# First three attention steps skewed by one level with their decays on VectorE, and each later step prepared one group earlier

## The reference

```python
def _attn_ref(q, k, v, alpha):            # (4, 8, 768, 48) each
    for t in range(S):
        state = alpha[:, :, t, :, None] * state + einsum('bhd,bhe->bhde', k[:, :, t], v[:, :, t])
        y[:, :, t] = einsum('bhd,bhde->bhe', q[:, :, t], state)
def _moe_ref(x, w_gate, w_val, w_out):    # x (3072, 384), d_ff 1536
    return (sigmoid(x @ w_gate) * (x @ w_val)) @ w_out
def _moe2_ref(x, domain_probs, w1, w2):   # 4 experts, F 1024
    p = domain_probs / (domain_probs.sum(-1, keepdims=True) + 1e-09)
    out = sum over e of p[:, e:e + 1] * (maximum(x @ w1[e], 0) @ w2[e])
```

## Time and profile before

| | |
|---|---|
| median of 3 runs | 1492.99 us (1491.99 to 1493.7) |
| profiled execution | 1493.83 us, span 1492.0 us |
| TensorE busy | 1438.6 us, 96% of the span |
| VectorE, ScalarE, GpSimd busy | 620.4, 501.0, 597.8 us |
| first dense matmul | 65.81 us after the span's start |

### The profile page before, as it was taken

One profiled execution on the slowest core, in us unless ns is written; L12 is line 12 of the kernel. 1 busy time (PEld: TensorE's weight loads), 2 busy tenths in 40 slices (PEclk: granted clock), 3 DMA queues, 4 the chain that ended last, 5 costly groups with the idle time before them and its releaser, 6 DMA issues.

```text
span 1492.0 us, 25792 instructions
## 1 busy us (share of the span) xinstructions
PE 1438.6 (96%) x10296; PEld 1327.3 (89%) x10296; DVE 620.4 (42%) x908; ACT 501.0 (34%) x975; POOL 597.8 (40%) x570
## 2 busy tenths in 40 slices
PE   3799999999999999999999999999999999999999
PEld 3688999898999898999999999999999999999998
DVE  8766654646455555312333333333333333333332
ACT  5554444545445445322222222222222222222220
POOL 7666454544444535254423413323234133242120
PEclk9999999999999999999999999999999999999999
DMA  6512122112121212100001001010010010100011
GB/s 229 188 51 102 51 84 70 68 67 70 66 88 52 93 60 83 43 22 22 0 1 43 0 1 43 0 43 1 1 42 0 0 42 0 42 0 0 19 44 63
DMA packets 31115, 70.70 MB, mean 47 GB/s; under 512 B 5168, under 2 KB 14128, under 8 KB 31024
## 3 DMA queue, kind: packets, MB, share of 16 engines
q1 hardware_dynamic: 31024, 69.43, 13.6%
HBM read 64.70 MB, written 4.72 MB: 47 GB/s over the span
## 4 chain that ended last, share of the span: by engine, by line
PE 89%; DVE 5%; issue 2%; POOL 2%; ACT 1%; DMA 1%; SPq 0%; DVEq 0%; ACTq 0%; POOLq 0%
PE PS L637 27%; PE PS L627 27%; PE PS L583 19%; PE PS L593 9%; PE PS L531 3%; PE PS L554 1%; DVE KQ L861 1%; PE PS L550 1%; ACT QX L738 1%; PE PS L534 1%; DVE near L866 1%; DMA V<-in_v 1%; DVE KQ L846 1%; DVE TOT L855 1%; DMA KQ<-in_qk 0%
## 5 line engine op out<-in xcount | busy, mean ns | idle before, releaser
L1094 POOL TENSOR_TENSOR XS_0l<-x2T,XS_0h 128x1536 fp32r<-128x1536 f32 x24 | 84.4, 3516 | 261.5 <-ACT XS_0h L781 261.5
L985 DVE SCALAR_TENSOR_TENSOR acc<-PS,prob,acc 128x384 f32<-128x384 f32 x192 | 118.7, 618 | 160.5 <-PE PS L637 160.5
L1094 POOL TENSOR_TENSOR XS_1l<-x2T,XS_1h 128x1536 fp32r<-128x1536 f32 x23 | 80.7, 3509 | 250.6 <-ACT XS_1h L781 250.6
L738 ACT ACTIVATE QX<-KQ 48x256 f32<-48x256 f32 x288 | 120.8, 419 | 139.5 <-DVE KQ L846 102.9
L820 ACT ACTIVATE H_1h<-PS 128x512 fp32r<-128x512 f32 x96 | 57.4, 598 | 309.9 <-PE PS L627 309.9
L820 ACT ACTIVATE H_0h<-PS 128x512 fp32r<-128x512 f32 x96 | 57.2, 598 | 297.3 <-PE PS L627 297.2
L846 DVE TENSOR_TENSOR KQ<-KQ,TOT 112x512 f32<-112x512 f32 (+1 forms) x144 | 126.9, 891 | 66.2 <-PE PS L531 37.7
L993 DVE SCALAR_TENSOR_TENSOR H_1l<-PS,H_1h 128x512 fp32r<-128x512 f32 x96 | 66.4, 691 | 195.8 <-ACT H_1h L820 195.8
L993 DVE SCALAR_TENSOR_TENSOR H_0l<-PS,H_0h 128x512 fp32r<-128x512 f32 x96 | 66.1, 691 | 187.4 <-ACT H_0h L820 187.4
L531 PE MATMUL PS<-QX,KQ 112*64 112x64 f32 x1920 | 86.7, 237 | 41.2 <-ACT QX L738 36.2
L531 PEld LDWEIGHTS PS<-QX,KQ 112*64 112x64 f32 x1920 | 73.2, 148 | 56.8 <-issue 27.9
(11 more groups left out here) (152 smaller groups left out, 4137.1 us busy)
## 6 DMA issues: line engine op xcount, KB each, us to landing
row<-in_rows SPq DMA_DIRECT2D x24, 768.0 KB, 4.3
KQ<-in_qk SPq DMA_DIRECT2D x24, 448.0 KB, 4.1
V<-in_v SPq DMA_DIRECT2D x24, 384.0 KB, 4.8
rawA<-in_w SPq DMA_DIRECT2D x8, 768.0 KB, 4.8
rawB<-in_w SPq DMA_DIRECT2D x8, 768.0 KB, 6.4
A<-in_alpha SPq DMA_DIRECT2D x24, 224.0 KB, 2.7
out_y<-acc SPq DMA_DIRECT2D x5, 768.0 KB, 3.5
raw<-in_w_gate SPq DMA_DIRECT2D x3, 768.0 KB, 8.4
```

The source lines that it names most:

```text
L738: done = nc.scalar.activation(QX[p][rows, :, g, :].rearrange("d a (n t) -> d a n t", t=2 << level), right, ACT.Copy)
L985: dve.scalar_tensor_tensor(out=acc[:, n, :], in0=PS[:, result_banks[u], 0:DM], scalar=weight, in1=acc[:, n, :], op0=ALU.mult, op1=ALU.add) ...
L1094: nc.gpsimd.tensor_tensor(XS[c % 2][1][:], x2T[:, :, at:at + T2], XS[c % 2][0][:].bitcast(F32), ALU.subtract).then_inc(xsl_ready, 1)
```

## The change

It does five things.

1. `FIRST` is a wave: step 1 runs one level behind step 0, and step 2 one behind step 1; before, all three ran the same level in turn.
2. The decays of these three steps are made by VectorE (`first_decays`, a `tensor_reduce` with multiplication over pairs, after each level) in PSUM banks 0, 1 and 2, which no one uses yet. GpSimd no longer makes them.
3. Steps 1 and 2 have row buffers of their own, so that all rows are loaded at the start; before, each load waited for the near terms of the step ahead.
4. The work on weight pieces moves: the low parts of pieces 3 to 5 are made by VectorE in tile 0, in ten parts, one behind each of the groups 0 to 9; the preparation of step 3 stands in slot 0 of tile 0.
5. In the slot tables a step's PREP stands two slots ahead of its level 0, not one, and in tile 0 all attention tasks stand two slots later.

The core of the diff, the tables and their use:

```diff
     def at(n):
-        return (n + lead) * ATT_GROUPS // count
+        return 2 + 2 * (n + lead) if first_tile else n * ATT_GROUPS // (4 * STEPS_T)
+    if first_tile:
+        slots[0].append((PREP, 0, 0))
...
             if 0 <= level < LEVELS:
                 tasks.append((LVL, j, level))
             if level == 0:
-                slots[at(n) - 1].append((PREP, j, 0))
+                slots[at(n) - 2].append((PREP, j, 0))
...
-FIRST = [(LVL, j, n) for n in range(LEVELS) for j in range(STEPS_T)]
...
+for n in range(LEVELS + STEPS_T + 2):
+    FIRST += [(LVL, j, n - j) for j in range(STEPS_T) if 0 <= n - j < LEVELS]
+    for j in range(STEPS_T):
+        if n - j == LEVELS:
+            FIRST += [(YOUT, j, 0), (STATE, j, 0)]
+        if n - j == LEVELS - 1:
+            FIRST.append((TRK, j, 0))
+        if n - j == LEVELS + 1:
+            FIRST.append((TRX, j, 0))
...
+        def tot_of(i, sc, h):
+            if not is_first(i, sc):
+                return TOT[buffer_of(i, sc)][h]
+            at = 2 * PAIRS * (HC - C // h)
+            return PS[:, sc, at:at + PAIRS * C // h].rearrange("r (a m) -> r a m", a=PAIRS)
...
+            def first_decays(sc, n):
+                if n:
+                    dve.wait_ge(*decays_done(0, sc, n))
+                tot = tot_of(0, sc, 2 << n)[0:R].rearrange("p a (n w) -> p a n w", w=2)
+                dve.tensor_reduce(tot_of(0, sc, 4 << n)[0:R], tot, AX.X, ALU.mult).then_inc(first_decay[sc], 1)
...
-            for j in range(STEPS_T):
-                decays(0, j)
             near_products(0, 0)
+            near_products(0, 1)
+            low_raw1(0)
             near_terms(0, 0)
-            low_raw1(0)
-            near_products(0, 1)
+            near_terms(0, 1)
+            near_products(0, 2)
             low_raw1(1)
...
             low_raw1(2)
+            near_terms(0, 2)
             near_products(0, STEPS_T)
-            decays(0, STEPS_T)
```

More of the change, by code:

```diff
@@ L275, in attention_moe_program @@
         row = sb("row", [P, 4, DM])
-        near = sb("near", [P, 2, H])
+        near = [sb(f"near{p}", [P, 2, H]) for p in range(2)]
         y_near = [sb(f"y_near{p}", [P, DM]) for p in range(2)]
@@ L289, in attention_moe_program @@
         WV = [sb(f"WV{c}", [P, KD, F1], F32R) for c in "hl"]
+        last_third = [top[0] + (n * FC1 + FC1 - THIRD) * DM * 4 for n in range(2)]
         WO = [sb(f"WO{c}", [P, FC1, DM], F32R) for c in "hl"]
+        first_rows = [row] + [nc.alloc_sbuf_tensor_at(f"row{n + 1}", [P, 4, DM], F32, offset=at) for n, at in enumerate(last_third)]
         xT = [[sb(f"xT0{c}", [P, KD, T1], F32R) for c in "hl"]]
@@ L321, in attention_moe_program @@
         rows_in = sem("rows_in")
+        first_rows_in = [sem(f"first_rows_in{j}") for j in range(STEPS_T)]
+        first_decay = [sem(f"first_decay{j}") for j in range(STEPS_T)]
         tot2_ready = sem("tot2_ready")
@@ L472, in _ @@
             load_rows(0, 0)
+            load_rows(0, 1)
             for n in range(len(pieces)):
@@ L888, in task @@
                     dve.wait_ge(level_done[p], per_level(i, sc, level))
-                    move_on(p, 2 << level, k_too=not (last and chunk == CHUNKS - 1), q_too=not (last and chunk == 0))
+                    move_on(i, sc, 2 << level, k_too=not (last and chunk == CHUNKS - 1), q_too=not (last and chunk == 0))
                     if level < MASKED:
@@ L929, in group, with tile @@
                     dve.tensor_tensor(hid[f % 2][:], PS[:, value_bank, 0:T1], hid[f % 2][:], ALU.mult).then_inc(h_ready, 1)
-            def tile(i, tc, attend=True, follow=True):
+            def tile(i, tc, attend=True, follow=True, between={}):
                 slots = slots_of(i, tc) if attend else []
@@ L946, in _ @@
             nc.vector.memset(PS[:, att_bank0:att_bank0 + ATT_BANKS, :], 0.0)
-            for j in range(STEPS_T):
-                prepare(0, j, 0)
-                prepare(0, j, 1)
+            prepare(0, 0, 0)
+            prepare(0, 0, 1)
+            prepare(0, 1, 0)
+            prepare(0, 1, 1)
             dve.wait_ge(mask_in, 16)
             dve.wait_ge(at_clear, 1)
-            after = {(LVL, 2, 0): (near_sums, 0, 0), (LVL, 2, 3): (near_sums, 0, 1), (YOUT, 1, 0): (near_sums, 0, 2),
-                     (LVL, 2, 5): (low_raw1, 3), (STATE, 1, 0): (low_raw1, 4)}
+            sums_after = {(LVL, 0, 3): 0, (LVL, 0, 4): 1, (STATE, 0, 0): 2}
             for t in FIRST:
                 task(0, 0, *t)
-                if t in after:
-                    after[t][0](*after[t][1:])
-            prepare(0, STEPS_T, 0)
-            prepare(0, STEPS_T, 1)
-            low_raw1(5)
+                if t == (LVL, 0, 0):
+                    prepare(0, 2, 0)
+                    prepare(0, 2, 1)
+                if t in sums_after:
+                    near_sums(0, sums_after[t])
             group(0, 0, "value", 0)
-            tile(0, 0)
+            parts = [(n, k) for n in (3, 4, 5) for k in range(THIRD if n == 5 else KD)]
+            tile(0, 0, between={at: (lambda n=n, k=k: low_part1(n, k)) for at, (n, k) in enumerate(parts)})
             dve.wait_ge(prob_in, 16)
```

91 lines of the change are left out of this document (50 added, 41 removed).

## The result

The changed kernel takes 1500.46 us (median of 11 runs, 1496.53 to 1502.14) against 1492.99 us (11 runs, 1491.23 to 1495.61) for the kernel before: the ratio is 1.0046, with a 95% interval of 1.0035 to 1.0056. It is slower, by 7.5 us. Its profiled execution took 1501.16 us, with a span of 1499.0 us against 1492.0 us.

A forecast was written before the change was run, and what follows sets the result against it. The start was taken as bound by a chain through other engines, the tiles by TensorE with holes. -11.8 - 1.0 + 17.0 + 3.0 + 6.2 = +13.4 us on 1493.83 gave 1507.2, less 0.8 to the median: 1506 us, range 1490 to 1518.

The forecast's parts named there:

- The mechanism named for it: Tiles: ScalarE copies the next step's columns, which wait for the preparation, before the running step's, stalling TensorE ahead of level 4.
- The start: Before the gated layer: first dense matmul at 54 us (50 to 58) instead of 65.8, a gain of 11.8 us.
- the signs: Listed checks: first dense matmul 50 to 58 us, moves never over 0.8, reduces 0.15 to 0.4, 17 waits before level 4.
- the start gains little: Start: slow reduces, slow moves or a late first weight piece put the first dense matmul at 60 us; 1513 us, chance 0.15.
- The first half clock: Behind the first dense matmul: the 3.8 us half-clock stretch, 1.9 us lost, goes with one chance in two; 1.0 us gained.
- Tile 0: First tile: later level-3 moves +0.8, step 3's preparation +0.7, low weights +1.0, last transpose +0.5; together +3.0 us.
- The tiles: After tile 0: longer stalls at six slots 0 (1.6 us), five slots 20 (1.4), six slots 10 (0.1); +17.0 us.
- The clock: Tiles: half-clock stretches of 3.4 us behind 2/6 of 17 long stalls, 1.7 us lost each; +6.2 us.
- no more half clock: Tiles: a stall ahead of both level products may keep the clock up; 1500 us, chance 0.22 for 1490 to 1502.
- the stalls do not grow: Tiles: ScalarE's level-4 copy is not late, slot 10's six stalls vanish; 1470 us, chance 0.12 for all below 1490.
- turning point: Tiles: the added cost for each of 17 preparations, clock included, at which the change turns from gain to loss: 0.58 us.

The follow-up runs named there:

- the start alone: The change with each preparation one slot ahead again, as in the kernel before, the rest kept: 1483.88 us, ratio 0.9949.
- the 32-byte shift: The kernel before plus an unused tile of 32 bytes a partition ahead of the weights: 1498.68 us (kernel before, beside it, 1492.82).
- the 64-byte kernel: The kernel before plus one unused pad tile of 64 bytes a partition, where the change has its second near tile: 1497.32 us, ratio 1.0032.
- the table alone: The kernel before with each preparation two slots ahead instead of one, all else as it was: 1508.53 us, ratio 1.0123.

## Why the prediction was right, and where its sizes were off

The forecast was "slower", at 1506 us; it is slower, at 1500.5. The mechanism named for it is the one that decides. That the forecast is only 6 us off is in part luck: the start won 2.1 us more than its term, the tiles and their clock cost 9.4 us less than theirs, and against that stand 1.0 us that the first stretch at half clock did not give back and 4.0 us in the experts, for which the sum had no term.

**The start: -11.8, measured -13.9.** The first dense matmul came at 51.9 us, inside 50 to 58. The moves (0.62 us from start to start in the sum, a duration of 0.67 us with overlap in the trace) and the reduces (4.1 us, measured 4.5) were sized rightly, though the first reduce of a step takes 0.46 to 0.47 us, over the 0.4 us of the signs. The sum was for 55 us, or 50 us "if the clock is up by then"; the row 45.00 to 51.90 has the granted clock at 1.00, so the second end was the nearer one. The rival "the start gains little" is out: neither the moves nor the reduces were slow. Of its conditions one came true in part: ScalarE waited 1.2 us for the first weight piece, and the chain of work that the profile follows back from the first dense matmul leads to that piece.

The Trainium skill ("SBUF — State Buffer", the section on the two sides of SBUF) says that GpSimd and a VectorE operation with two SBUF inputs take a shared pair of ports by an exclusive lock, the loser waiting out the whole instruction. The run with the decays in SBUF agrees: 3.47 us beside a subtraction of 3.43 us, 0.69 us without one.

**The first half clock: -1.0, measured about nothing.** TensorE's last wait became 1.28 us, as supposed, and a 3.4 us stretch at half clock stood behind the first dense matmul all the same (3.8 us before).

**Tile 0: +3.0, measured +3.0** (95.6 against 92.6 us). The parts are less good than the sum. I had its long stalls stay at about 1.7 us; three of them are 2.1 to 2.3 us. At the first, ScalarE's copies begin at 77.30 us, 0.4 us after TensorE had run dry, and take 1.75 us. With the order set right the change's tile 0 lasts 91.0 us (142.1 - 51.1), so the order costs 4.6 us here.

**The tiles: +17.0, measured +13.8.** The place, the number and the length of the stalls were right: 17, in front of level 4, 1.5 to 1.8 us each, 28.5 us of waits where 28 was forecast. What was too large, by 3.2 us, is the step from a stall to its cost. At slots 0 and 20 I took all of the later start of level 4 as loss. But in the kernel before the row of 32 level products lasts 1.46 us and in the change 1.15 us: before, the second half of that row still waited inside for the copies of level 0, and the row hides it. Both columns are there when TensorE resumes in the change, so 0.3 us come back at each of eleven slots: 6 x 1.3 + 5 x 1.1 = 13.3 us, and slot 10 gives 1.71 + 1.15 against 0.69 + 1.52 + 0.69, nothing. That is 0.5 us from the measured 13.8.

**The clock: +6.2, measured 0.** This is the step that was wrong. It took the rate of the kernel before, two stretches at half clock for six long stalls, and multiplied it by 17; the change had two for 17. The rival "no more half clock" gave 1500 us for this case, because the stall stands in front of two level products and not between them, and the traces side with it. Five kernels have the stall between the products in their six tiles: 12 stretches at half clock behind 30 long stalls (two each in the kernel before, the start alone and the 32-byte shift, three each with 64 and 128 bytes; those of the 64-byte kernel stand below). Three kernels have it in front: 4 behind 51 (two in the change, two in the change with `near1` moved, none in the table alone).

```profile
186.90:190.30 3.40, 3.40 (x11) 3.40 (x12) 1.92 (x2) 1.85 (x5) 3.24 (x5) 0.50 0.02 5
...
507.80:511.20 3.40, 3.40 (x12) 3.40 (x11) 1.09 (x1) 1.24 (x3) 2.50 (x3) 0.50 0.00 0
```

So the rate itself was no bad guess for stalls of the old form; it was carried to another form. Each count is one trace a kernel, and kernels of one form have nearly the same timing, so the cases are not independent. And the form is not all of it: in tile 0 all three kernels with the stall in front have two stretches for the three stalls at a preparation, which are longer there (2.1 to 3.4 us). What decides in a single case stays open.

**The experts: no term, measured +4.0.** No part of the prediction looked at what else the second `near` buffer does. Six kernels with the 64-byte shift have 802.9 to 803.0 us there, the pad alone brings it about, and moving the 64 bytes to the end takes it away in two kernels. Without it the change is at 1495.5 us.

So the numbers close: -13.9 + 3.0 + 13.8 + 0.1 + 4.0 = +7.0 of span. The rival on the other side, "the stalls do not grow", gave 1470 us, and the kernel with ScalarE's two passes in the other order is that case: 1470.6 us, with the experts' 4 us still in it and a start 2 us better than its sum had. Its turning point was 0.58 us for each of 17 preparations, clock included; the measured 13.8 us of the tiles are 0.81 each.

## What to carry to other kernels

When work is moved ahead in a table that several engines read, look at each in-order queue for what now stands behind the moved piece: a copy that isn't needed for two groups, placed in front of one that is due, cost over 25 us here, and issuing the urgent copies first made the whole change a gain. Take the loss from the instruction behind the stall too, since what follows a late start is often ready and runs closer. And when a change adds a buffer, however small, see what lies behind it: compare the matmuls per 100 us of a stage that the change leaves alone.

## What the runs showed of the hardware

- TensorE's rate in the expert stage depends on where its tiles lie in SBUF. With the region shifted by 0 and 128 bytes a partition the expert stage took 798.3 to 798.9 us, by 32 bytes 802.1 us, by 64 bytes 802.9 to 803.0 us, at a granted clock of 1.00 with TensorE idle for 2.9 to 3.0 us of the stage in each. At 64 bytes some groups of matmuls take up to 6 ns more (396 against 390 ns) and others, of tiles that moved together, the same 389 ns. Which tiles have to lie how was not tried; the 32 and 128 byte cases are one run each.
- A VectorE product with one input in PSUM is not slower than one with both in SBUF: 0.68 and 0.69 us for 512 columns of 112 partitions, 0.54 and 0.55 us for 384. Beside GpSimd it is on average half as long, 0.67 against 1.26 us.
- Stalls of TensorE of 1.5 to 1.9 us can be followed, 0.7 to 1.7 us after work resumes, by a stretch of 3.4 us at 1.2 instead of 2.4 GHz. In the six tiles 12 of 30 were where the stall stood between two level products, 4 of 51 where it stood in front of both.
